# Another order of the attention turns, and of the crossing into the next block, on four engines of a three-block kernel

## The reference, cut to what matters

```python
def sm_attn(qq, kk, vv):                      # softmax attention, scale 1/8
    s = scale * np.matmul(qq, kk.transpose(0, 1, 3, 2))
    s = s - np.max(s, axis=-1, keepdims=True)
    a = np.exp(s)
    a = a / (np.sum(a, axis=-1, keepdims=True) + 1e-09)
    return np.matmul(a, vv)
p_packed = sm_attn(p, k, v)                   # 8 batches x 8 heads, p 32 x 64, k and v 576 x 64
out = sm_attn(q, p_packed, p_packed)          # q 576 x 64
# then, on 4608 tokens x 512:
#   h = x @ w_in (512 x 2048); g = P(h) / Q(h), a rational function; y = g @ w_out
#   h = y @ w_in2 (512 x 1024); a softmax-weighted layer norm; out = ... @ w_out2
```

## Time and profile before

| what | value |
|---|---|
| time, median of 3 runs | 1224.36 us (1224.18 to 1226.65) |
| the profiled execution's own time | 1224.68 us |
| its span, first to last instruction | 1222.8 us |
| mean granted TensorE clock | 0.98 |
| busy: PE | 1160.7 us (95%) |
| busy: DVE | 1057.4 us (86%) |
| busy: ACT | 834.9 us (68%) |
| busy: POOL | 436.3 us (36%) |
| chain of work that ended last | PE 84%, DVE 12%, issue 2%, ACT 1% |

### The profile page before, as it was taken

One profiled execution on the slowest core, in us unless ns is written; L12 is line 12 of the kernel. 1 busy time (PEld: TensorE's weight loads), 2 busy tenths in 40 slices (PEclk: granted clock), 3 DMA queues, 4 the chain that ended last, 5 costly groups with the idle time before them and its releaser, 6 DMA issues.

```text
span 1222.8 us, 23134 instructions
## 1 busy us (share of the span) xinstructions
PE 1160.7 (95%) x8736; PEld 1029.3 (84%) x8736; DVE 1057.4 (86%) x1686; ACT 834.9 (68%) x1334; POOL 436.3 (36%) x284
## 2 busy tenths in 40 slices
PE   5688778999999999999999999999999999999998
PEld 3344446999999999999999999987888888888887
DVE  5877879999999999999999999988687776776763
ACT  4466669888888888888888888845455454454543
POOL 2343323334243342433433333354344354343300
PEclk9878989999999999999999999999999999999999
DMA  9988856021210212202122021131121111211211
GB/s 343 334 315 295 309 189 254 31 79 47 75 62 28 81 47 72 64 28 81 48 72 64 28 82 38 55 106 30 40 62 43 51 43 43 55 48 35 60 26 35
DMA packets 72799, 116.13 MB, mean 95 GB/s; under 512 B 9728, under 2 KB 40448, under 8 KB 72704
## 3 DMA queue, kind: packets, MB, share of 16 engines
q1 hardware_dynamic: 72704, 114.85, 28.9%
HBM read 74.46 MB, written 40.37 MB: 94 GB/s over the span
## 4 chain that ended last, share of the span: by engine, by line
PE 84%; DVE 12%; issue 2%; ACT 1%; DMA 0%; SPq 0%; ACTq 0%; DVEq 0%
PE ps_y L73 11%; PE ps_y L75 11%; PE ps_y L74 11%; PE ps_h L73 6%; PE ps_h L75 6%; PE ps_h L74 6%; PE ps_o L73 5%; PE ps_o L75 5%; PE ps_o L74 5%; PE ps_h L1441 4%; PE ps_h L1442 4%; PE ps_h L1443 4%; PE ps_t L1466 2%; PE ps_s L457 2%; DVE kT L634 2%
## 5 line engine op out<-in xcount | busy, mean ns | idle before, releaser
L1065 POOL TENSOR_TENSOR den<-den,h_abs 128x576 f32<-128x576 f32 x128 | 222.0, 1734 | 403.9 <-ACT den L1018 403.9
L73 PE MATMUL ps_y<-g_hi,wout_hi 128*128 128x288 f32 x1024 | 303.2, 296 | 0.0
L74 PE MATMUL ps_y<-g_lo,wout_hi 128*128 128x288 f32 x1024 | 302.1, 295 | 0.0
L75 PE MATMUL ps_y<-g_hi,wout_lo 128*128 128x288 f32 x1024 | 301.1, 294 | 0.0
L75 PEld LDWEIGHTS ps_y<-g_hi,wout_lo 128*128 128x128 f32 x1024 | 192.9, 188 | 0.0
L74 PEld LDWEIGHTS ps_y<-g_lo,wout_hi 128*128 128x128 f32 x1024 | 192.1, 188 | 0.0
L73 PEld LDWEIGHTS ps_y<-g_hi,wout_hi 128*128 128x128 f32 x1024 | 191.8, 187 | 0.3 <-ACT wp_out L565 0.2
L73 PE MATMUL ps_h<-x_hi,wp_hi 128*128 128x288 f32 x512 | 153.2, 299 | 0.7 <-DVE num L1096 0.5
L74 PE MATMUL ps_h<-x_lo,wp_hi 128*128 128x288 f32 x512 | 151.9, 297 | 0.0
L75 PE MATMUL ps_h<-x_hi,wp_lo 128*128 128x288 f32 x512 | 151.3, 295 | 0.0
L1012 ACT ACTIVATE h_abs<-ps_h 128x576 f32<-128x576 f32 x128 | 83.3, 651 | 84.0 <-PE ps_h L75 83.8
(11 more groups left out here) (168 smaller groups left out, 2568.2 us busy)
## 6 DMA issues: line engine op xcount, KB each, us to landing
wp_scratch<-wp_out SPq DMA_DIRECT2D x32, 512.0 KB, 3.8
wp_lo<-wp_scratch SPq DMA_DIRECT2D x32, 512.0 KB, 4.1
k_main<-in_k SPq DMA_DIRECT2D x16, 576.0 KB, 6.7
q_main<-in_q SPq DMA_DIRECT2D x16, 576.0 KB, 6.3
v_main<-in_v SPq DMA_DIRECT2D x16, 576.0 KB, 7.2
y_scratch<-y_out SPq DMA_DIRECT2D x16, 576.0 KB, 3.4
y_lo<-y_scratch SPq DMA_DIRECT2D x36, 256.0 KB, 3.3
out<-result SPq DMA_DIRECT2D x144, 64.0 KB, 1.7
```

The source lines that it names most:

```text
L73: pe.matmul(out, lh, rh, start=first, stop=False)
L74: pe.matmul(out, lh, rl, start=False, stop=False)
L75: return pe.matmul(out, ll, rh, start=False, stop=last)
L1065: pool.tensor_tensor(den[s % 3][:, :, :], den[s % 3][:, :, :], h_abs[:, :, :], ALU.mult)\
```

## The change

The same instructions are issued, except that `pack` is no longer cut in two, that `row_max` is cut into `row_max` (L640) and `shift1` (the four L643 and L647), and that `turn_queries` gives its first transpose to `turn_last_queries`. All else is the order of the lists.

- PE: `pack` in one piece; then the transpose of the last pair of q, `turn_packed`, the other eight transposes of q, `scores_of_q`, both job blocks, `scores_of_packed`.
- DVE: `inverse_sum1` before `row_max`, `normalized_pack` and `second_sums` between `row_max` and `shift1`, `packT_low` and `turn_probs2` behind it, `turn_keys` late.
- ACT: `second_terms(i-2)` at the start of the turn, then `packT_to_sbuf(i-1)` and `weights_high`, and only then `first_terms(i)`.
- SP: the job's store behind the load of v, and the load of q behind that.
- Behind the last turn: other orders on PE, ACT, DVE, and on POOL `normalized_probs2` of the last but one group ahead of the first two steps.

```diff
--- before.py
+++ after.py
@@ -337,8 +337,6 @@
         load_q(sp, 1)
 
         for i in range(GROUPS - 1):
-            if i >= 1 and job_at(i - 1) is not None:
-                store_job(sp, job_at(i - 1))
             if i + 2 < GROUPS:
                 sp.wait_ge(kT_ready, i + 1)
                 load_k(sp, i + 2)
@@ -346,16 +344,19 @@
                 load_p(sp, i + 2)
                 for n in w_loads(i):
                     load_w(sp, n)
-                sp.wait_ge(qT_done, i + 1)
-                load_q(sp, i + 2)
             else:
                 first_chunk(sp)
             wait_for(sp, pack_done, i)
             load_v(sp, i + 1)
+            if i >= 1 and job_at(i - 1) is not None:
+                store_job(sp, job_at(i - 1))
+            if i + 2 < GROUPS:
+                sp.wait_ge(qT_done, i + 1)
+                load_q(sp, i + 2)
+            else:
+                first_block(sp)
             if i == 0:
                 coefficients(sp)
-            if i + 2 == GROUPS:
-                first_block(sp)
             if i >= 2:
                 store_a2(sp, i - 2)
 
@@ -409,37 +410,40 @@
                                        start=(b == 0), stop=(b == DB - 1), skip_group_check=True)
             mm.then_inc(s1_done, 1)
 
-        def pack(pe, i, half):
-            if half == 0:
-                if i == 0:
-                    pe.wait_ge(same_row_ready, 1)
...
-            if half == 1:
-                mm.then_inc(pack_done, 1)
-
-        def turn_queries(pe, i):
+            mm.then_inc(pack_done, 1)
+
+        def q_pair(i, j):
+            return q_main[i % 2][:, 2 * j:2 * j + 2, :].rearrange("p t d -> p (t d)")
+
+        def turn_last_queries(pe, i):
             pe.wait_ge(q_in[i % 2], 16 * (i // 2 + 1))
             if i == 0:
                 pe.wait_ge(consts, 1)
...
+            pe.transpose(turn_q8, q_pair(i, PAIRS - 1), ident[:, :]).then_inc(qT8_done, 1)
+
+        def turn_queries(pe, i):
             wait_for(pe, qT_out, i)
-            wait_for(pe, wp_act_out, 2 * jobs_before(i))
-            pair = lambda j: q_main[i % 2][:, 2 * j:2 * j + 2, :].rearrange("p t d -> p (t d)")
-            pe.transpose(turn_q8, pair(PAIRS - 1), ident[:, :]).then_inc(qT8_done, 1)
             for j in range(PAIRS - 1):
-                mm = pe.transpose(turn_q[:, j // 4, j % 4 * P:(j % 4 + 1) * P], pair(j), ident[:, :])
+                mm = pe.transpose(turn_q[:, j // 4, j % 4 * P:(j % 4 + 1) * P], q_pair(i, j), ident[:, :])
             mm.then_inc(qT_done, 1)
 
         def turn_packed(pe, i):
@@ -478,41 +482,38 @@
         scores_of_packed(pe, 0)
         for i in range(GROUPS):
             if i >= 1:
-                pack(pe, i - 1, 0)
+                pack(pe, i - 1)
+            turn_last_queries(pe, i)
+            if i >= 1:
+                turn_packed(pe, i - 1)
             turn_queries(pe, i)
             if i >= 1:
-                pack(pe, i - 1, 1)
+                scores_of_q(pe, i - 1)
             job_block(pe, i, 0)
-            if i >= 1:
-                turn_packed(pe, i - 1)
             job_block(pe, i, 1)
-            if i == GROUPS - 1:
-                pe.wait_ge(exp1_ready, GROUPS)
-                features(pe, 0)
-            if i >= 1:
-                scores_of_q(pe, i - 1)
             if i + 1 < GROUPS:
                 scores_of_packed(pe, i + 1)
 
         last = GROUPS - 1
         b, c, d, e, f = range(JOBS - LAST_JOBS, JOBS)
+        pack(pe, last)
         last_block(pe, b, 0)
-        pe.wait_ge(wp_act_out, 2 * (b - 1) + 1)
-        features(pe, 1)
-        pack(pe, last, 0)
-        pack(pe, last, 1)
         turn_packed(pe, last)
         last_block(pe, b, 1)
+        pe.wait_ge(exp1_ready, GROUPS)
+        features(pe, 0)
+        last_block(pe, c, 0)
         scores_of_q(pe, last)
+        last_block(pe, c, 1)
+        features(pe, 1)
         features(pe, 2)
-        last_block(pe, c, 0)
-        last_block(pe, c, 1)
         last_block(pe, d, 0)
         last_block(pe, d, 1)
+        last_block(pe, e, 0)
         features(pe, 3)
-        for m in (e, f):
-            for n in range(2):
-                last_block(pe, m, n)
+        last_block(pe, e, 1)
+        last_block(pe, f, 0)
+        last_block(pe, f, 1)
 
     def scalar(act, next_coefficients, early):
         act.preload_act_table_set("natural_log_exp_and_others")
@@ -567,59 +568,57 @@
         for i in range(GROUPS - 1):
             if i == 3:
                 next_coefficients(act)
-            first_terms(act, i)
-            if len(parts_at(i)) > 1:
-                weights_high(act, parts_at(i)[0])
-            last_pair_to_sbuf(act, i)
-            qT_to_sbuf(act, i)
-            if len(parts_at(i)) == 1:
-                weights_high(act, parts_at(i)[0])
+            if i >= 2:
+                second_terms(act, i - 2)
             if i == 1:
                 act.wait_ge(zeros, 1)
             if i >= 1:
                 packT_to_sbuf(act, i - 1)
+                for n in parts_at(i):
+                    weights_high(act, n)
+            first_terms(act, i)
+            last_pair_to_sbuf(act, i)
+            qT_to_sbuf(act, i)
+            if i == 0:
+                weights_high(act, 0)
             if job_at(i) is not None:
                 job_to_sbuf(act, job_at(i), 0)
                 job_to_sbuf(act, job_at(i), 1)
-            if len(parts_at(i)) > 1:
-                weights_high(act, parts_at(i)[1])
-            if i >= 1:
-                second_terms(act, i - 1)
 
         last = GROUPS - 1
         a, b, c, d, e, f = range(job_at(last), JOBS)
-        early["x_hi"](act, 0)
-        early["block_hi"](act, 0)
+        second_terms(act, last - 2)
+        packT_to_sbuf(act, last - 1)
         first_terms(act, last)
         last_pair_to_sbuf(act, last)
         qT_to_sbuf(act, last)
-        packT_to_sbuf(act, last - 1)
+        early["x_hi"](act, 0)
         job_to_sbuf(act, a, 0)
         job_to_sbuf(act, a, 1)
+        early["block_hi"](act, 0)
+        job_to_sbuf(act, b, 0)
+        second_terms(act, last - 1)
+        packT_to_sbuf(act, last)
+        job_to_sbuf(act, b, 1)
         act.wait_ge(w_lo_done, GROUPS)
         early["head"](act, 0)
-        job_to_sbuf(act, b, 0)
-        second_terms(act, last - 1)
-        act.wait_ge(probs1T_ready, GROUPS)
+        early["block_hi"](act, 1)
+        job_to_sbuf(act, c, 0)
+        early["reciprocal"](act, 0)
+        early["block_hi"](act, 2)
         early["head"](act, 1)
-        packT_to_sbuf(act, last)
-        early["block_hi"](act, 1)
-        job_to_sbuf(act, b, 1)
-        early["reciprocal"](act, 0)
+        second_terms(act, last)
+        job_to_sbuf(act, c, 1)
+        job_to_sbuf(act, d, 0)
+        early["head"](act, 2)
+        job_to_sbuf(act, d, 1)
+        job_to_sbuf(act, e, 0)
         early["reciprocal"](act, 1)
-        early["head"](act, 2)
-        job_to_sbuf(act, c, 0)
-        job_to_sbuf(act, c, 1)
-        early["block_hi"](act, 2)
-        job_to_sbuf(act, d, 0)
-        job_to_sbuf(act, d, 1)
-        second_terms(act, last)
         early["head"](act, 3)
-        job_to_sbuf(act, e, 0)
         job_to_sbuf(act, e, 1)
-        early["reciprocal"](act, 2)
         job_to_sbuf(act, f, 0)
         job_to_sbuf(act, f, 1)
+        early["reciprocal"](act, 2)
 
     def vector(dve, next_coefficients, early):
         dve.memset(packT2[:, :, :], 0.0).then_inc(zeros, 1)
@@ -638,6 +637,9 @@
         def row_max(dve, i):
             dve.wait_ge(s1_done, i + 1)
             dve.tensor_reduce(max1, scores1, AX.X, ALU.max).then_inc(max1_ready, 1)
+
+        def shift1(dve, i):
+
             dve.wait_ge(max1_ready, i + 1)
             for n in range(GH):
                 other = dve.tensor_scalar(other1[head(n ^ 1), :], max1[head(n), :], -ATT_SCALE, None, ALU.mult)
@@ -704,56 +706,59 @@
         for i in range(GROUPS - 1):
             if i == 3:
                 next_coefficients(dve)
+            if i >= 1:
+                inverse_sum1(dve, i - 1)
             row_max(dve, i)
-            turn_keys(dve, i + 1)
+            if i >= 1:
+                normalized_pack(dve, i - 1)
             if i >= 2:
                 second_sums(dve, i - 2)
+            shift1(dve, i)
             if i >= 1:
-                inverse_sum1(dve, i - 1)
-                normalized_pack(dve, i - 1)
-            turn_probs1(dve, i)
+                packT_low(dve, i - 1)
             if i >= 2:
                 turn_probs2(dve, i - 2)
-            if i >= 1:
-                packT_low(dve, i - 1)
+            turn_keys(dve, i + 1)
+            turn_probs1(dve, i)
             if i >= 1:
                 shifted_scores(dve, i - 1)
 
         last = GROUPS - 1
+        inverse_sum1(dve, last - 1)
         row_max(dve, last)
+        normalized_pack(dve, last - 1)
         second_sums(dve, last - 2)
...
     def gpsimd(pool, step):
 
@@ -777,12 +782,12 @@
                 normalized_probs2(pool, i - 2)
             for n in parts_at(i):
```

(62 more changed lines are left out.)

## The result

The changed kernel took 1257.88 us in the median of 4 runs (1252.26 to 1262.56), the kernel before, on the same chip, 1224.54 (4 runs, 1224.18 to 1226.65): ratio 1.027, 95% interval 1.021 to 1.032. Slower, as forecast, but by 33 us where 10.6 were forecast, and above the range. The profiled execution took 1254.37, span 1252.5, mean granted clock 0.963.

What follows compares the result with a forecast made beforehand. DVE was taken to bound turns 2 to 14. 10 turns x 12.2 + 3 x 10.2 = 152.6 against 139.14 gave +13.5, with the crossing's -3 +10.5: forecast 1235 us, range 1209 to 1247, the forecast's own 1224 to 1248.

Steps and rivals of the forecast that it cites:

- DVE bounds the turn: Turns 2 to 14: DVE's own work sets the turn, 9.11 us before and 8.9 after the change.
- The crossing's waits: Inside each turn, DVE's two waits, for ACT's high part and PE's scores of q, go: -0.98 us per full-clock turn.
- Loss 1: shift1 behind second_sums: the second small L643 waits out POOL's L767, 0.90 us per turn, between 0 and 1.16.
- Loss 2: weights_high earlier on ACT: L647 waits out POOL's low part of the weight, 2.2 us per turn, between 0 and 2.37.
- SP's moves: Store of a job and load of q behind the load of v, k's load late: hidden, cost 0.
- starts within 0.1 of L649: Sign of a stalled turn: POOL's low part at 3.10, just before DVE's last shift1 instruction at 3.13.
- Rival 1: In the turns, DVE's last shift1 instruction starts before POOL's low part: turns 9.8, kernel 1213 us; chance 0.32.
- and I add 0.2 for job blocks and scores at the lower clock: Stalled turns: 0.2 us on top of 12.0, as some PE work at the lower clock outlasts DVE.
- done at 9.4 of a turn of 9.8: PE's list in a turn: pack ends at 9.4 of 9.8 us, so PE is not what is late next.
- at 26% of the time that is 3 of 13 turns: Turns 2 to 14: a lower-clock transpose delays POOL's low part, so 3 turns escape the 2.2 stall, at 10.2 us.
- the 12.2 forecast: Length of each of 10 stalled turns: 8.9 + 0.9 + 2.2 = 12.0, plus 0.2 for the lower clock.
- the crossing: Crossing into the rational layer, behind the last turn: new lists gain, -3 us, between -6 and +4.

Runs made afterwards that it cites:

- e6: Changed kernel with shift1 ahead of second_sums, turn_keys ahead of turn_probs2 on DVE, and ACT's weights_high behind the copies of q: 1202.01 us, ratio 0.982.
- e3: Changed kernel with 20 more identity transposes on PE in turns 1 to 13, while it waits for packT_low: 1240.44 us, ratio 1.014.
- e7: Changed kernel with SP's order of before in turns 0 to 14: 1253.42 us, ratio 1.024.
- e10: Changed kernel with two one-column copies into unused memory on ACT ahead of weights_high: 1216.08 us, ratio 0.995.
- e4: Kernel before, all turns up to 14 as before, with the changed kernel's lists from the last turn on: 1222.05 us, ratio 0.997.
- e1: Changed kernel with shift1 put back ahead of second_sums on DVE: 1215.75 us, ratio 0.991.
- e2: Changed kernel with ACT's weights_high put back behind the copies of q: 1219.39 us, ratio 0.995.

## Why the prediction was right, and where it failed

*Right.* DVE bounds the turn with 8.9 us of its own: 8.93 in e6, 12.0 less 3.1 in e3. The crossing's waits vanish: no idle time ahead of L681. Loss 1: forecast 0.90 on top of 0.16, measured 1.049 to 1.052 for the second L645 in all 13 turns. The first starts 0.02 behind the end of L695 (128.93 against 128.64 + 0.27), so it is held behind it as the prediction took it to be. Loss 2: forecast 2.2 on top of 0.16, measured 2.27 in all, 2.1 on top, in 12 of 13 turns. SP's moves: forecast 0, measured 0 (e7). That POOL's low part (L778, before L773) starts within 0.1 of L649 and decides the sign was right too. Counted from L667, POOL starts at 3.08 and L649 at 3.16, where 3.10 and 3.13 were forecast, the same to 0.02 in all 12 stalled turns; that was worked out and not luck. Rival 1's turn was 9.8, and e10's full-clock turn is 9.87 at 1216 us against its 1213.

*The steps that failed.* First, "and I add 0.2 for job blocks and scores at the lower clock": the measured term is 1.64 in a settled turn (13.64 against 12.0). The prediction gives no working for the 0.2, and it knows the lower clock only as the share of before, with PE's waits of before. But the stall makes a wait of its own, 3.72 us, and the job blocks and scores behind it, 120.89 to 125.90 in the turn shown, run at the lower clock; with PE kept busy in that wait they do not (e3). The scores (L407) end 6.69 us behind L649 here and 4.60 behind it in e3, 2.1 us more. The prediction gave PE's list 0.4 us of slack at full clock ("done at 9.4 of a turn of 9.8").

Second, "at 26% of the time that is 3 of 13 turns": one turn escaped. The mechanism was right (L451 at 0.48, then L649 first), the frequency was not. A clock share averaged over a turn says nothing about one instruction: in the settled turn L451 comes behind `pack` and the first transpose of q and takes 0.33 each time, while the lower clock lies elsewhere.

The balance: the 12 stalled turns take 168.36 - 10.80 = 157.56, 13.13 each, 0.93 more than the 12.2 forecast: 11.2 us. Two turns more than forecast stall, 2.0 each: 4.0. The one that escaped took 10.8, not 10.2: 0.6. Together 15.8, which is 168.4 - 152.6.

Third, the crossing: forecast -3, measured -1.3 alone (e4) and +1.1 in the changed kernel, whose crossing still begins with a stalled turn's 1.27 us wait for the sum (of L658, at 194.35). The largest gain was e1's, 2.0: a gain of at most two thirds of the forecast. Over the whole kernel the profiled execution lies 19.2 above the forecast's 1235.2: 15.8 from the turns and 4.1 from the crossing, less the 0.8 that turns 0 and 1 gained, which the forecast put at 0, and little else.

*What stays open.* The changed kernel's executions spread over 10 us, 1252.26 to 1262.56; only one was profiled, so how many turns escape in the others is not known. Nor was it tried why turns 6 and 7 are shorter than the settled 13.6, or why single later turns are long (13.25 in e1). Of loss 1 it is not shown why L645, with one tensor input, is held at all.

## What to carry to other kernels

Before moving tiny VectorE instructions, look at what GpSimd runs beside them in the new order: one of two elements can cost as much as GpSimd's longest. Where a forecast adds a stall to a turn, follow the engine that starves behind it and price its work at the clock that this wait leaves it, not at the average of before. Where two chains reach a shared point within 0.05 us, state the sign as a toss, and look for the small delay that decides it.

## What the runs showed of the hardware that was not expected

- The order of two starts decides: a scalar_tensor_tensor that starts 0.06 us ahead of GpSimd's instruction takes 0.16, one that starts 0.07 to 0.09 behind it takes 2.27. With 0.2 us more work on ScalarE (e10) the kernel goes from 1257.9 to 1216.1.
- The price is what is left of GpSimd's instruction, not a matter of the VectorE instruction's size. Two elements end within 0.02 of GpSimd's end, and the subtraction of 128 x 576 (L683) 0.61 to 0.62 behind it: 1.23 with 0.61 left and 1.76 with 1.15 left (e2), 2.16 with 1.54 left (before). The other way round GpSimd pays: its subtraction that starts 0.11 behind L683 in turn 6 of e6 takes 2.87 by the profile, the others of that run 2.35 to 2.37. Of the four small tensor_scalar only the one that follows GpSimd's start waits; the first was already running.
- The kernel before pays it in its last block too: L1749, the instruction of the earlier trace rows, started 0.02 to 0.03 behind a GpSimd instruction in 16 of its 18 executions and took 1.27 to 1.29 in each; in the other two, with none beside it, 0.16.
- Transposes of the identity that nobody reads made the kernel faster (e3), by 11 us in turns 2 to 14: the mean clock in turns 2 to 14 went from 0.77 to 0.96, and the settled turn from 13.64 to 12.0.
